# The low halves of the first layer's weights: a ScalarE write and an adding transfer in place of a VectorE subtraction

## The chip, the core and the metric

One Trainium2 chip, one of its cores. The metric is the device time in microseconds (us) of one launch. The core has TensorE (matrix products), VectorE and ScalarE (elementwise work), GpSimd (elementwise work, and the issue of indirect and adding transfers), SyncE (here it only issues transfers) and 16 DMA engines that all queues share. Each engine has its own instruction stream and runs it in order; a semaphore wait in it holds up everything behind it.

## The reference, cut to what matters

Attention over chunks gives `x` of 3072 tokens by 512. Then come two layers of eight experts, each with weights `w1` (512 x 1024) and `w2` (1024 x 512) in float32:

```python
def _moe_ref(x, w_gate, w1, w2):            # first layer
    cap = N // E                            # 384 tokens for each expert
    order = np.argsort(-(x @ w_gate).flatten())
    ...                                     # best pairs first; an expert closes when it has cap tokens
    for e in range(E):
        mask = assigned == e
        h = np.maximum(x[mask] @ w1[e], 0.0)
        out[mask] = h @ w2[e]

def _moe2_ref(x, w_gate, w_noise, noise, w1, w2):   # second layer
    ...                                     # two experts for each token, softmax over their two logits
    for e in range(E):
        for k in range(2):
            mask = top2[:, k] == e
            h = np.maximum(x[mask] @ w1[e], 0.0)
            out[mask] += top2_w[mask, k, None] * (h @ w2[e])
```

## The kernel before

TensorE multiplies operands of type fp32r, which keep fewer bits than float32. So each factor is split in two: a high half, the value rounded to fp32r, and a low half, value minus high half, rounded too. A product is the sum of three passes, high x high, high x low and low x high (`PASSES`). Weights are split in the core: `w1_sb` and `w2_sb` hold the raw weights of one expert, `w1_part[0]`, `w2_part[0]` the high halves and `[1]` the low halves.

An expert's weights are cut into eight parts `c` of 512 KB, four of `w1` (0 to 3) and four of `w2` (`CH` + 0 to `CH` + 3, that is 4 to 7). For each part and each turn (0 to 7: the eight experts of the first layer; 8, called E: the first expert of the second layer; from 9 on: the tiles of the second) four things happen:

- SyncE loads the raw part (`load_weights`, L474; in the second layer L495) once the low half of the part's previous turn has been written (`lo_ready`).
- ScalarE writes the high half (`w_high`, L530), when the raw part is there (`w_loaded`) and TensorE has finished with the part's last turn (`wait_used`).
- VectorE writes the low half (`w_low`, L536): `raw - high`, 128 x 1024 elements.
- TensorE waits for `hi_ready` and `lo_ready` ahead of the first product that uses the part (L726, L747).

There is one raw buffer, so the next load of a part waits for the low half.

The launch has four stages. Attention lasts to about 230 us. In the first expert layer (230 to 686 us) step `n` chooses the tokens of the `n`-th expert to be filled (a search in seven rounds `s` for a threshold: VectorE compares, L1115; TensorE counts, L682 and L689; VectorE reads the count, L1143 and L1164), and in its gaps the code written out by hand runs the experts before: for `k = n - 1` the token numbers are worked out (L1068 to L1071), GpSimd gathers its 384 rows (`xg`, three indirect transfers, L356, then three of noise, L360), TensorE transposes them (`turn_xg`, L696) and does its first products (`hidden`, L730); for `j = n - 2` TensorE does the rest of `hidden` and the second products (`combine`, L750), ScalarE copies the result out (`copy_y`, L1446) for a store and a transpose (`turn_y`, L704). Steps 0 to 6 choose; steps 7, 8 and 9 only finish the experts left. A routing stage (686 to 729 us) is a chain of small VectorE instructions that plans the second layer. The second layer runs 29 tiles of 256 rows to the end.

The order on ScalarE in a step is: the last `s1_high` (L1435) of the step before, `w_high` of parts 6 and 7, two `s1_high`, `w_high` 0 and 1, `copy_y` 0, `w_high` 2 and 3, `copy_y` 1, the copies of `xg`, `w_high` 4, `copy_y` 2, `w_high` 5, then `s1_high` of the next expert. VectorE's `w_low` stand at L1130 and L1159 (parts 6 and 7), L1139 and L1161 (0 to 3), L1184 and L1204 (4 and 5), and L1382 for turn E.

## Time and profile before

| | us |
|---|---|
| Median of 3 runs (lowest to highest) | 1428.52 (1428.26 to 1435.44) |
| The profiled execution, its own time | 1426.65 |
| Its span, first to last instruction | 1424.9 |
| Of that: first expert layer | about 230 to 686 |
| Routing stage | 686 to 729 |
| Second layer | 729 to the end |

Times in rows of the trace are microseconds from the start of the span. PE is TensorE (PEld its weight loads), DVE VectorE, ACT ScalarE, POOL GpSimd, SP SyncE. In a timeline, a row is start, duration, engine, line, operation, output and inputs, count, and in brackets the idle time before it with what ended it.

### The profile page before, as it was taken

The numbers are of one execution on the slowest core, as the hardware profiler recorded it, in microseconds if no ns is written. First come the engines' busy times: TensorE is split into PE (matmuls) and PEld (weight loads), VectorE is DVE, ScalarE is ACT, GpSimd is POOL, SyncE is SP. The second block draws the span as 40 slices with busy tenths as digits, with TensorE's granted clock in tenths as the row PEclk, the third lists the DMA queues.
The fourth block names the chain that finished last, engine by engine and source line by source line (L and its number), as shares of the span: only waits on it lengthen the run. The fifth ranks groups of instructions, "written<-read, shape, count | busy, mean of one in ns | idle before, by whom it ended". The sixth has DMA issues, their size and how long they took to land.

```text
span 1424.9 us, 28417 instructions
## 1 busy us (share of the span) xinstructions
PE 1268.4 (89%) x9825; PEld 1125.7 (79%) x9825; DVE 952.5 (67%) x1904; ACT 594.2 (42%) x1252; POOL 294.3 (21%) x345
## 2 busy tenths in 40 slices
PE   7999962599989999889249999999999999999997
PEld 6888851478778778768149999898989999999996
DVE  4777757788888787344666666666666666666662
ACT  4666621123323323333214545444445454444541
POOL 2000000210220210220122423332323333333322
PEclk9999975599999999899659999999999999999999
DMA  8888853133333233432013425124343324252110
GB/s 144 169 161 166 169 199 120 57 123 115 102 111 113 88 123 115 144 133 72 16 46 104 133 60 177 38 82 134 94 147 117 131 81 138 72 163 87 61 32 3
DMA packets 174760, 154.62 MB, mean 109 GB/s; under 512 B 105581, under 2 KB 138349, under 8 KB 174704
## 3 DMA queue, kind: packets, MB, share of 16 engines
q1 hardware_dynamic: 151552, 102.83, 26.2%
q0 software_dynamic: 16608, 44.56, 10.1%
q10 hardware_dynamic: 6544, 6.49, 1.3%
q8 instruction: 35, 0.57, 0.2%
q14 instruction: 21, 0.17, 0.0%
HBM read 215.58 MB, written 34.28 MB: 175 GB/s over the span
## 4 chain that ended last, share of the span: by engine, by line
issue 38%; PE 31%; DVE 12%; POOL 10%; DMA 6%; ACT 2%; POOLq 1%; DVEq 0%; SPq 0%; ACTq 0%
PE bank L730 6%; PE bank L750 5%; POOL partial L400 3%; DMA out<-result,token_now 3%; PE bank L612 3%; POOL out L404 3%; DMA xg<-x_dram,token_of 3%; PE bank L621 2%; PE bank L600 2%; POOL held L382 2%; PE bank L682 2%; POOL x L386 2%; PE bank L636 2%; PE bank L696 1%; PE bank L629 1%
## 5 line engine op out<-in xcount | busy, mean ns | idle before, releaser
L536 DVE TENSOR_TENSOR w_part<-w_sb,w_part 128x1024 fp32r<-128x1024 f32 x296 | 361.1, 1223 | 113.8 <-ACT w_part L530 105.4
L530 ACT CAST w_part<-w_sb 128x1024 fp32r<-128x1024 f32 x296 | 307.0, 1046 | 215.1 <-PE bank L890 169.7
L873 PEld LDWEIGHTS bank<-x2T,w_part 128*128 128x128 f32 x2784 | 339.2, 193 | 4.0 <-DVE x2T L1332 1.8
L873 PE MATMUL bank<-x2T,w_part 128*128 128x256 f32 x2784 | 340.1, 284 | 1.4 <-DVE x2T L1332 1.4
L890 PE MATMUL bank<-w_part,h2T 128*128 128x512 f32 x1392 | 323.2, 391 | 0.0
L890 PEld LDWEIGHTS bank<-w_part,h2T 128*128 128x128 f32 x1392 | 259.2, 188 | 52.6
L750 PE MATMUL bank<-w_part,hT 128*128 128x512 f32 x576 | 155.3, 409 | 8.2 <-DVE w_part L536 8.2
L730 PE MATMUL bank<-xgT,w_part 128*128 128x384 f32 x768 | 146.4, 345 | 2.6 <-DVE hT L1040 1.8
L356 POOL DMA_INDIRECT xg<-x_dram,token_of x24 | 32.6, 1358 | 554.9 <-DVE token_of L1071 302.5
L1544 ACT ACTIVATE h2T<-bank 128x512 fp32r<-128x512 f32 x116 | 69.3, 597 | 174.8 <-PE bank L873 174.8
L730 PEld LDWEIGHTS bank<-xgT,w_part 128*128 128x128 f32 x768 | 135.8, 192 | 5.0 <-DVE hT L1040 1.6
L1338 DVE SCALAR_TENSOR_TENSOR h2T<-bank,h2T 128x512 fp32r<-128x512 f32 x116 | 80.2, 692 | 86.0 <-ACT h2T L1544 86.0
L750 PEld LDWEIGHTS bank<-w_part,hT 128*128 128x128 f32 x576 | 103.4, 190 | 28.1 <-issue 9.7
L382 POOL TENSOR_TENSOR held<-iota_p 1x1 f32<-1x1 f32 x87 | 41.3, 475 | 406.7 <-DVE result L1357 388.3
L1392 ACT ACTIVATE probs<-bank,neg_max 96x128 f32<-96x128 f32 x256 | 89.3, 368 | 7.9 <-DVE neg_max L909 7.9
L1435 ACT ACTIVATE hT<-bank 128x384 fp32r<-128x384 f32 x64 | 31.5, 492 | 126.6 <-PE bank L730 126.6
L1357 DVE SCALAR_TENSOR_TENSOR result<-bank,w_now,partial 128x512 f32<-128x512 f32 x58 | 43.4, 748 | 44.8 <-PE bank L890 44.8
L386 POOL DMA_INDIRECT x<-y_dram,slot_now x58 | 60.9, 1050 | 56.0 <-DVE slot_now L1324 38.6
L682 PEld LDWEIGHTS bank<-above,proposal 128*8 128x8 bf16 x1176 | 31.8, 83 | 51.1 <-DVE above L1115 44.1
L682 PE MATMUL bank<-above,proposal 128*8 128x32 bf16 (+1 forms) x1176 | 37.5, 177 | 38.8 <-DVE above L1115 38.8
L400 POOL DMA_INDIRECT partial<-out,token_now x58 | 62.5, 1078 | 18.6 <-issue 16.2
L404 POOL DMA_INDIRECT out<-result,token_now x58 | 59.2, 1021 | 21.6 <-POOL held L382 16.0
(256 smaller groups left out, 1341.9 us busy)
## 6 DMA issues: line engine op xcount, KB each, us to landing
w_sb<-in_moe_w SPq DMA_DIRECT2D x296, 512.0 KB
k_in<-in_k SPq DMA_DIRECT2D x32, 240.0 KB
v_in<-in_v SPq DMA_DIRECT2D x32, 240.0 KB
q_in<-in_q SPq DMA_DIRECT2D x32, 192.0 KB
x_dram<-x_sb SPq DMA_DIRECT2D x32, 192.0 KB, 3.4
out<-zeros SPq DMA_DIRECT2D x1, 6144.0 KB, 19.7
y_dram<-y_sb ACTq DMA_DIRECT2D x24, 256.0 KB, 2.0
x<-y_dram,slot_now POOLq DMA_INDIRECT x58
```

Source lines behind the costliest of these rows:

```text
L386: pool.indirect_dma_start(out=x2[:, par, half, :], out_offset=None, in_=y_dram[:, :], in_offset=bass.IndirectOffsetOnAxis(ap=slot_now[:, p ...
L400: pool.indirect_dma_start(out=partial[:, par, half, :], out_offset=None, in_=out[:, :], in_offset=tokens[half], bounds_check=N - 1, oob_is ...
L404: pool.indirect_dma_start(out=out[:, :], out_offset=tokens[half], in_=result[:, par, half, :], in_offset=None, bounds_check=N - 1, oob_is_ ...
L530: scalar.copy(split_part(0, c), raw_part(c)).then_inc(hi_ready[c], 1)
L536: nc.vector.tensor_tensor(split_part(1, c), raw_part(c), split_part(0, c).bitcast(F32), ALU.subtract).then_inc(lo_ready[c], 1)
L682: last = nc.tensor.matmul(counts[:, 0:bins], proposal[:, c, :], above[:, c, 0:bins], start=(c == 0), stop=(c == COLS - 1))
L730: last = nc.tensor.matmul(bank[2 + f % 2][:, 0:CAP], w1_part[a][:, kt, f * P:(f + 1) * P], xgT[b][:, kt, :], start=(kt == 0 and n == 0), s ...
L750: last = nc.tensor.matmul(bank[4 + t % 2][:, :], hT[a_][:, f, t * P:(t + 1) * P], w2_part[b_][:, f, :], start=(f == 0 and n == 0), stop=(f ...
L873: last = nc.tensor.matmul(bank[2 + g % 2][:, at:at + TILE], w1_part[a][:, kt, f * P:(f + 1) * P], x2T[b][:, kt, :], start=(f % 2 == 0 and ...
L890: last = nc.tensor.matmul(bank[4 + half][:, :], h2T[a][:, f, half * P:(half + 1) * P], w2_part[b][:, f, :], start=(f == 0 and n == 0), sto ...
L1338: V.scalar_tensor_tensor(h2T[1][:, two_f, :].rearrange("p k s -> p (k s)"), bank[2 + g % 2][:], 0.0, h2T[0][:, two_f, :].bitcast(F32).rear ...
L1392: nc.scalar.activation(probs[:, r, j, :], ps_s[r][0:QB, j * P:(j + 1) * P], ACT.Exp, bias=neg_max[:, r, j:j + 1], accum_out=row_sum[:, i % ...
```

## The change

For turns 0 to E, thus for 9 x 8 = 72 parts, VectorE's subtraction is gone. ScalarE writes, right behind each high half, the negated high half by multiplying the raw part by -1.0 with the low-half tile of type fp32r as output (the same rounding, other sign; `minus_ready`). GpSimd then issues a transfer from the raw tile to the low-half tile that adds (`w_low_add`, `accum_op=ALU.add`; `lo_added`). So the tile ends as raw minus high, as before. The loads of SyncE and the products of TensorE wait for `lo_added`. In GpSimd's stream the adds of parts 0 to 3 of turn `e` stand ahead of the gathers of expert `e`, those of parts 4 to 7 behind its noise gathers; for turn E they stand behind the loop and behind the two clears of `x2` and `partial`. The second layer's other turns keep VectorE's subtraction; its counts now start from 0, so that the first of the tiles is told apart (`reload`, `wait_low`). The helpers `wait_used`, `raw_part`, `split_part`, `w_high` and `w_low` are moved up in the file, unchanged but for the lines below. Blank lines are left out here.

```diff
@@ -284,6 +284,8 @@
         o_done = sem("o_done")
         token_ready = sem("token_ready")
         hi_ready = [sem(f"hi_ready{c}") for c in range(2 * CH)]
+        minus_ready = [sem(f"minus_ready{c}") for c in range(2 * CH)]
+        lo_added = [sem(f"lo_added{c}") for c in range(2 * CH)]
         lo_ready = [sem(f"lo_ready{c}") for c in range(2 * CH)]
         part_used = [sem(f"part_used{c}") for c in range(2 * CH - 1)]
         h_hi = sem("h_hi")
@@ -299,6 +301,43 @@
 
             eng.wait_ge(tiles_ready, 1)
             return eng.value_load(pairs_i[0:1, 0:1], min_val=2 * N // TILE // 2 - 1, max_val=(TILES - 3) // 2)
+        FC = F // CH
+        def wait_used(eng, turn, c, layer):
+            if isinstance(turn, int) and turn == 0:
+                return
+            if c < 2 * CH - 1:
+                eng.wait_ge(part_used[c], turn)
+            elif layer == 1:
+                eng.wait_ge(y_ready, TPE * turn)
+            else:
+                eng.wait_ge(o_ready, 2 * (turn - E))
+        def raw_part(c):
+            return w1_sb[:, :, c * FC:(c + 1) * FC] if c < CH else w2_sb[:, (c - CH) * FC // P:(c - CH + 1) * FC // P, :]
+        def split_part(side, c):
+            return w1_part[side][:, :, c * FC:(c + 1) * FC] if c < CH else w2_part[side][:, (c - CH) * FC // P:(c - CH + 1) * FC // P, :]
+        def w_high(turn, c, layer):
+            scalar = nc.scalar
+            scalar.wait_ge(w_loaded[c], 16 * (turn + 1))
+            wait_used(scalar, turn, c, layer)
+            scalar.copy(split_part(0, c), raw_part(c)).then_inc(hi_ready[c], 1)
+            if layer == 1:
+                scalar.mul(split_part(1, c), raw_part(c), -1.0).then_inc(minus_ready[c], 1)
+        def w_low(turn, c, layer):
+            wait_used(nc.vector, turn, c, layer)
+            nc.vector.wait_ge(hi_ready[c], turn + 1)
+            nc.vector.tensor_tensor(split_part(1, c), raw_part(c), split_part(0, c).bitcast(F32), ALU.subtract).then_inc(lo_ready[c], 1)
+        def w_low_add(turn, c):
+            nc.gpsimd.wait_ge(minus_ready[c], turn + 1)
+            nc.gpsimd.dma_start(split_part(1, c), raw_part(c), accum_op=ALU.add).then_inc(lo_added[c], 16)
 
         @block.gpsimd
         def _(pool):
@@ -348,6 +387,8 @@
 
 
             for e in range(E):
+                for c in range(CH):
+                    w_low_add(e, c)
                 pool.wait_ge(tokens_ready, e + 1)
                 if e:
 
@@ -360,6 +401,10 @@
                     pool.indirect_dma_start(out=noise_g[:, c, :], out_offset=None, in_=moe2_noise[:, :],
                                             in_offset=bass.IndirectOffsetOnAxis(ap=token_of[:, c:c + 1], axis=0),
                                             bounds_check=N - 1, oob_is_err=False).then_inc(noise_in, 16)
+                for c in range(CH, 2 * CH):
+                    w_low_add(e, c)
+            for c in range(CH):
+                w_low_add(E, c)
 
 
             pool.wait_ge(g2_copied, E * TPE)
@@ -368,6 +413,8 @@
             nc.gpsimd.memset(x2[:], 0.0).then_inc(x2_cleared, 1)
             nc.gpsimd.memset(partial[:], 0.0).then_inc(x2_cleared, 1)
             pool.wait_ge(x2_cleared, 2)
+            for c in range(CH, 2 * CH):
+                w_low_add(E, c)
 
 
             pool.wait_ge(tiles_ready, 1)
@@ -469,7 +516,7 @@
             def load_weights(e, w1, w2, turn):
                 for c in range(2 * CH):
                     if not (isinstance(turn, int) and turn == 0):
-                        sp.wait_ge(lo_ready[c], turn)
+                        sp.wait_ge(lo_added[c], 16 * turn)
                     raw, src = weight_part(w1, w2, e, c)
                     sp.dma_start(raw, src).then_inc(w_loaded[c], 16)
 
@@ -486,13 +533,20 @@
 
             load_weights(0, moe2_w1, moe2_w2, E)
             sp.wait_ge(tiles_ready, 1)
-            with sp.Fori(1, 2 * tile_pairs(sp) + 3) as j:
+            def reload(j):
                 e = sp.value_load(expert_i[0:1, bass.ds(j, 1)], min_val=0, max_val=E - 1)
                 changed = sp.value_load(change_i[0:1, bass.ds(j, 1)], min_val=0, max_val=1)
                 for c in range(2 * CH):
-                    sp.wait_ge(lo_ready[c], E + j)
+                    if isinstance(j, int):
+                        sp.wait_ge(lo_added[c], 16 * (E + 1))
+                    else:
+                        sp.wait_ge(lo_ready[c], j - 1)
                     raw, src = weight_part(moe2_w1, moe2_w2, e, c)
                     sp.dma_start(raw, src, cond=changed).then_inc(w_loaded[c], 16)
+            reload(1)
+            with sp.Fori(2, 2 * tile_pairs(sp) + 3) as j:
+                reload(j)
 
         def tiles(eng, tile, pairs):
 
@@ -502,41 +556,6 @@
                 tile(2 * g + 2, 0, True, g + 1)
             tile(2 * pairs + 1, 1, True, pairs)
             tile(2 * pairs + 2, 0, False, pairs + 1)
...
         def expert_steps(eng, step):
             step(0, True, None, None)
@@ -724,7 +743,7 @@
                     pe.wait_ge(s1_lo, e * FT + f - 1)
                 if f % 2 == 0:
                     pe.wait_ge(hi_ready[f // 2], e + 1)
-                    pe.wait_ge(lo_ready[f // 2], e + 1)
+                    pe.wait_ge(lo_added[f // 2], 16 * (e + 1))
                 for kt in range(KT):
                     for n, (a, b) in enumerate(PASSES):
                         last = nc.tensor.matmul(bank[2 + f % 2][:, 0:CAP], w1_part[a][:, kt, f * P:(f + 1) * P], xgT[b][:, kt, :],
@@ -745,7 +764,7 @@
                         pe.wait_ge(s1_lo, e * FT + f + 1)
                         if f % 2 == 0:
                             pe.wait_ge(hi_ready[CH + f // 2], e + 1)
-                            pe.wait_ge(lo_ready[CH + f // 2], e + 1)
+                            pe.wait_ge(lo_added[CH + f // 2], 16 * (e + 1))
                     for n, (a_, b_) in enumerate(PASSES):
                         last = nc.tensor.matmul(bank[4 + t % 2][:, :], hT[a_][:, f, t * P:(t + 1) * P], w2_part[b_][:, f, :],
                                                 start=(f == 0 and n == 0), stop=(f == FT - 1 and n == 2))
@@ -858,6 +877,13 @@
                             last = nc.tensor.transpose(bank[pair][:, at:at + P], x2[:, par, half, kt * P:(kt + 1) * P], ident[:])
                     last.then_inc(x2_turned, 1)
 
+            def wait_low(j, c):
+                if isinstance(j, int) and j == 0:
+                    pe.wait_ge(lo_added[c], 16 * (E + 1))
+                else:
+                    pe.wait_ge(lo_ready[c], j)
             def tile(j, par, more, pair_no):
                 pe.wait_ge(x_lo, 2 * j + 2)
                 for g in range(CH):
@@ -865,7 +891,7 @@
 
                         pe.wait_ge(h_lo, CH * j + g - 1)
                     pe.wait_ge(hi_ready[g], E + j + 1)
-                    pe.wait_ge(lo_ready[g], E + j + 1)
+                    wait_low(j, g)
                     for f in (2 * g, 2 * g + 1):
                         at = (f % 2) * TILE
                         for kt in range(KT):
@@ -885,7 +911,7 @@
                         if half == 0 and f % 2 == 0:
                             pe.wait_ge(h_lo, CH * j + f // 2 + 1)
                             pe.wait_ge(hi_ready[CH + f // 2], E + j + 1)
-                            pe.wait_ge(lo_ready[CH + f // 2], E + j + 1)
+                            wait_low(j, CH + f // 2)
                         for n, (a, b) in enumerate(PASSES):
                             last = nc.tensor.matmul(bank[4 + half][:, :], h2T[a][:, f, half * P:(half + 1) * P], w2_part[b][:, f, :],
                                                     start=(f == 0 and n == 0), stop=(f == FT - 1 and n == 2))
@@ -1084,9 +1110,7 @@
                 link(V.tensor_scalar(fill_f[:], marked, -1.0, float(E), ALU.mult, ALU.add))
                 V.tensor_copy(fill_i[:, bass.ds(n, 1)], fill_f[:]).then_inc(fill_known, 1)
 
-            def step(n, route, k, j, wk=None):
-                if wk is None:
-                    wk = k
+            def step(n, route, k, j):
                 if route:
 
                     link(V.tensor_tensor(work[:], logits[:], over_cols(limit[:]), ALU.min))
@@ -1127,7 +1151,6 @@
                             s1_low(j, 5)
                         if s == 1:
                             s1_low(j, 6)
-                            w_low(j, CH + 2, 1)
                     if k is not None:
                         if s == 1:
                             taken_tiles(k)
@@ -1135,8 +1158,6 @@
                             taken_rows(k, 0)
                         if s == 6 and route:
                             xg_low(k, 1)
-                    if wk is not None and s in (3, 4, 5):
-                        w_low(wk, (0, 1, 3)[s - 3], 1)
                     if route:
                         dve.wait_ge(counts_up, n * len(SHIFTS) + s + 1)
 
@@ -1156,9 +1177,6 @@
                             xg_low(k, 2)
                     if j is not None and s == 1:
                         s1_low(j, 7)
-                        w_low(j, CH + 3, 1)
-                    if wk is not None and s == 4:
-                        w_low(wk, 2, 1)
                     if route:
                         dve.wait_ge(votes_up, n * len(SHIFTS) + s + 1)
                         link(V.tensor_scalar(votes[:, 1:bins], votes_ps[:, 1:bins], 1.0 if s == 0 else float(1 << shift), 0.0,
@@ -1181,7 +1199,6 @@
                 if k is not None:
                     for kt in (3,) if route else range(KT):
                         xg_low(k, kt)
-                    w_low(k, CH, 1)
                 if route:
 
                     dve.wait_ge(tally_up, n + 1)
@@ -1201,7 +1218,6 @@
                     link(V.scalar_tensor_tensor(room[:], filled[:], CLOSED, et[3][:], ALU.mult, ALU.add))
                     link(V.scalar_tensor_tensor(limit[:], filled[:], -3e38, limit[:], ALU.mult, ALU.add))
                 if k is not None:
-                    w_low(k, CH + 1, 1)
                     s1_low(k, 0)
                     s1_low(k, 1)
                 if route:
@@ -1238,7 +1254,7 @@
             step(E - 1, False, E - 2, E - 3)
             step(E, False, E - 1, E - 2)
 
-            step(E + 1, False, None, E - 1, E)
+            step(E + 1, False, None, E - 1)
 
 
             dve.wait_ge(g2_copied, E * TPE)
@@ -1378,8 +1394,6 @@
 
             for t in range(TPE):
                 dve.wait_ge(y_stored[t], 16 * E)
-            for c in range(CH, 2 * CH):
-                w_low(E, c, 1)
             meta(0, 0, 0, False)
             x_low(0)
             tiles(dve, tile, tile_pairs(dve))
```

## Rows read from the trace of the kernel before

**Rows 1.** Part 1 of the page: busy time and share of each engine.
```profile
PE 1268.4 (89%) x9825; PEld 1125.7 (79%) x9825; DVE 952.5 (67%) x1904; ACT 594.2 (42%) x1252; POOL 294.3 (21%) x345
```

**Rows 2.** Groups by line, 280 to 700 us: busy, mean ns, idle before.
```profile
L536 DVE TENSOR_TENSOR w_part<-w_sb,w_part 128x1024 fp32r<-128x1024 f32 x63 | 76.1, 1219 | 3.9 <-ACT w_part L530 3.1
L530 ACT CAST w_part<-w_sb 128x1024 fp32r<-128x1024 f32 x66 | 66.3, 1045 | 4.4 <-ACT y_sb L1446 4.4
```

**Rows 3.** Sums of waits, 280 to 700 us: total, times, longest.
```profile
PE bank L696 <- DMA xg<-x_dram,token_of: 8.6, 7, 2.3
PE bank L750 <- DVE w_part L536: 8.2, 8, 1.4
```

**Rows 4.** The chain that ended last, ends of one selection step: start, duration.
```profile
448.71 0.97 DVE above L1115
...
503.16 0.97 DVE above L1115
```

**Rows 5.** Timeline of TensorE, same step: start, duration, idle before.
```profile
458.90 1.55 PE L750 MATMUL bank<-w_part,hT 128*128 128x512 f32 x6
...
461.46 1.62 PE L750 MATMUL bank<-w_part,hT 128*128 128x512 f32 x6 [0.89 <-DVE w_part L536]
...
476.99 0.76 PE L682 MATMUL bank<-above,proposal 128*8 128x32 bf16 x24 [1.00 <-DVE above L1115]
478.76 0.54 PE L696 MATMUL bank<-ident,xg 128*128 128x128 f32 x3 [1.01 <-DMA xg<-x_dram,token_of]
...
488.92 0.66 PE L704 MATMUL bank<-ident,y_sb 128*128 128x128 f32 x4
```

**Rows 6.** Timeline of ScalarE, same step.
```profile
449.86 1.99 ACT L530 CAST w_part<-w_sb 128x1024 fp32r<-128x1024 f32 x2
...
459.48 1.98 ACT L530 CAST w_part<-w_sb 128x1024 fp32r<-128x1024 f32 x2
...
464.30 2.00 ACT L530 CAST w_part<-w_sb 128x1024 fp32r<-128x1024 f32 x2 [0.60 <-ACT y_sb L1446]
...
487.33 1.05 ACT L530 CAST w_part<-w_sb 128x1024 fp32r<-128x1024 f32 x1
488.28 0.59 ACT L1446 COPY y_sb<-bank 128x512 f32<-128x512 f32 x1
```

**Rows 7.** Timeline of VectorE, same step.
```profile
460.09 1.22 DVE L536 TENSOR_TENSOR w_part<-w_sb,w_part 128x1024 fp32r<-128x1024 f32 x1
```

**Rows 8.** Timeline of GpSimd, same step: issues of the first two gathers.
```profile
471.36 1.00 POOL L356 DMA_INDIRECT xg<-x_dram,token_of  x1 [44.34 <-DVE token_of L1071]
472.66 1.99 POOL L356 DMA_INDIRECT xg<-x_dram,token_of  x1 [0.30 <-issue]
```

**Rows 9.** Line 356 (gathers): issue to landing.
```profile
DMA to landing us min/median/max: 3.7/4.2/8.6
```

**Rows 10.** Stage 500 to 504 us: length, busy times, clock, DMA share, GB/s.
```profile
500.00:504.00 4.00, 3.88 (x24) 3.34 (x23) 3.76 (x9) 0.58 (x2) 0.00 (x0) 1.00 1.05 373
```

**Rows 11.** Timeline of TensorE, first step without a selection.
```profile
565.12 1.55 PE L750 MATMUL bank<-w_part,hT 128*128 128x512 f32 x6
568.03 2.96 PE L750 MATMUL bank<-w_part,hT 128*128 128x512 f32 x12 [1.35 <-DVE w_part L536]
...
584.34 0.55 PE L696 MATMUL bank<-ident,xg 128*128 128x128 f32 x3 [2.00 <-DMA xg<-x_dram,token_of]
```

**Rows 12.** Timeline of ScalarE, same step as rows 11.
```profile
558.76 1.99 ACT L530 CAST w_part<-w_sb 128x1024 fp32r<-128x1024 f32 x2
...
569.73 0.59 ACT L1446 COPY y_sb<-bank 128x512 f32<-128x512 f32 x1 [2.03 <-PE bank L750]
```

**Rows 13.** Timeline of VectorE, start of the second layer.
```profile
728.64 4.63 DVE L536 TENSOR_TENSOR w_part<-w_sb,w_part 128x1024 fp32r<-128x1024 f32 x4
```

**Rows 14.** Timeline of GpSimd, start of the second layer: second gather.
```profile
731.05 1.96 POOL L386 DMA_INDIRECT x<-y_dram,slot_now  x1 [0.30 <-issue]
```

**Rows 15.** Timeline of TensorE, start of the second layer.
```profile
735.48 1.97 PE L858 MATMUL bank<-ident,x 128*128 128x128 f32 x8 [8.58 <-DMA x<-y_dram,slot_now]
```

More of the change, by code:

```diff
@@ L504, in tiles @@
             tile(2 * pairs + 2, 0, False, pairs + 1)
-        FC = F // CH
-        def wait_used(eng, turn, c, layer):
-            if isinstance(turn, int) and turn == 0:
-                return
-            if c < 2 * CH - 1:
-                eng.wait_ge(part_used[c], turn)
-            elif layer == 1:
-                eng.wait_ge(y_ready, TPE * turn)
-            else:
-                eng.wait_ge(o_ready, 2 * (turn - E))
-        def raw_part(c):
-            return w1_sb[:, :, c * FC:(c + 1) * FC] if c < CH else w2_sb[:, (c - CH) * FC // P:(c - CH + 1) * FC // P, :]
-        def split_part(side, c):
-            return w1_part[side][:, :, c * FC:(c + 1) * FC] if c < CH else w2_part[side][:, (c - CH) * FC // P:(c - CH + 1) * FC // P, :]
-        def w_high(turn, c, layer):
-            scalar = nc.scalar
-            scalar.wait_ge(w_loaded[c], 16 * (turn + 1))
-            wait_used(scalar, turn, c, layer)
-            scalar.copy(split_part(0, c), raw_part(c)).then_inc(hi_ready[c], 1)
-        def w_low(turn, c, layer):
-            wait_used(nc.vector, turn, c, layer)
-            nc.vector.wait_ge(hi_ready[c], turn + 1)
-            nc.vector.tensor_tensor(split_part(1, c), raw_part(c), split_part(0, c).bitcast(F32), ALU.subtract).then_inc(lo_ready[c], 1)
         def expert_steps(eng, step):
```

## Prediction

> **What bounds the kernel now.** I read part 1 of the page first [rows 1]: TensorE is busy for 89% of the span, VectorE for 67%. The change touches only the first expert layer and the two seams behind it, so the rest is left alone; the groups and sums of waits from 280 to 700 us come next [rows 2, 3]. VectorE's low halves cost 1.22 us each, and of the 63 in that stretch only 8 had TensorE waiting, 8.2 us in all. The gathers of `xg` made it wait as long: 8.6 us. So the 72 removed instructions (72 x 1.22 = 88 us of VectorE) are not 88 us of the end. A selection step lasts 54.45 us [rows 4], and its TensorE timeline shows three gaps near this work [rows 5]: 0.89 us ahead of the products at 461.46, for the low half of part 7; 1.00 us ahead of the count at 476.99, for a compare that VectorE reached late; 1.01 us ahead of the transposes at 478.76, for the gathers. TensorE is nearly full and the gathers are the next limit. What the step can win is under 3 us, and what the step can lose is whatever makes part 6, part 7 or the gathers later.
>
> **What goes away.** VectorE's low half of part 7 ran from 460.09 [rows 7] and its end freed TensorE. Without it the products need only `s1_low`, and could start 0.9 us sooner, if the added half is there. In the steps without selection the gap is 1.35 us [rows 11]. The late compare (1.00 us) also goes, but behind it TensorE meets the gathers in order, so that gap moves into the wait for them. It is worth something only if the gathers come sooner. They could: the second gather's issue took 1.99 us where the first took 1.00 [rows 8], at the same time as low halves on VectorE, and the same is seen where the second layer starts: 1.96 us [rows 14] during four low halves in a row [rows 13].
>
> The Trainium skill, page SBUF — State Buffer, section "Who interferes with whom", says that a VectorE instruction with two SBUF inputs contends with a GpSimd instruction that reads SBUF. By that the longer issues are those under the subtractions, as seen here; the sum is the same without it.
>
> **What ScalarE adds.** 72 multiplications of the size of the cast, which takes 1.045 us [rows 2]: 75 us on an engine with much room. A multiplication of this shape is not in the trace; below, nothing of its size is cheaper than 0.59 us for 512 columns [rows 6], above, I see no reason for more than the cast. I take 1.0 us. Most lie in idle time. One place does not: `copy_y` 2 stands directly behind `w_high` 4, at 488.28 for 0.59 us, and TensorE's transpose that needs it starts at 488.92 with no gap [rows 5, 6]. One more microsecond ahead of it is a microsecond of TensorE: +0.95 us in each of the five steps that select and finish an expert (steps 2 to 6). In steps 7 and 8 `copy_y` 2 comes ahead of `w_high` 4, cost nothing there.
>
> **What an add costs.** No add is in the trace. It moves 524,288 bytes. Weight loads, at full share of the DMA engines, move 373 GB/s [rows 10]: 1.4 us for a part. An add must read the raw half and the tile and write the tile. From below: 1.4 us, if both reads overlap. From above: nothing bounds an adder's rate, so I take twice the doubled load, 5.6 us. The value taken is two reads at the load's rate, 2.8 us. Around it: a gather of 256 KB takes 3.7 us from issue to landing [rows 9], of which 0.7 us is data at 373 GB/s, so 3.0 us is fixed; the release of GpSimd costs some 0.7 us (the gathers' token numbers against the issue at 471.36 [rows 8]). An add lands about 0.7 + 3.0 + 2.8 = 6.5 us after its minus half, and adds in a row land 2.8 us apart.
>
> The Trainium skill, page Collectives: The Full Stack, section "The bandwidth ceiling: the fold count and why AG ≠ RS ≠ AR", says that an adding transfer needs two source reads on the same ring and so runs at half the rate of a copy, not because the adder costs cycles. By that an add is 2.8 us of data, as taken, and the 5.6 us bound would be out; no row here shows it.
>
> The issue itself: GpSimd spends 1.00 us on a gather of 128 rows [rows 8]. A part of `w2` is 128 contiguous runs of 4 KB, so I take 1.0 us. A part of `w1` is 512 runs of 1 KB: from below 1.0 us, from above four times, 4.0 us. I take 2 us, as part of a gather's microsecond is fixed.
>
> **Parts 6 and 7.** High halves 6 and 7 start at 449.86 [rows 6]; with a minus half behind each, minus 6 ends near 451.9 and minus 7 near 453.9. Add 6 lands at 458.4; TensorE needs it at 458.90 [rows 5]. Add 7 lands at 461.2, or 461.9 with the load of part 6 beside it; now the products start at 461.46. So the 0.9 us is not won: +0.5 us instead. In step 7 the pair starts at 558.76 [rows 12], minus 6 ends at 560.8, add 6 lands at 567.3, needed at 565.12; add 7 lands at 570.1 against 568.03 now [rows 11]: about +2.2 us, likewise in steps 8 and 9.
>
> **Parts 0 to 3 against the gathers.** The pair at 459.48 becomes four instructions to 463.5; `copy_y` 0 and then the pair now at 464.30 follow, so minus 3 ends near 468.6 [rows 6]. Add 0 starts to move at about 463.2; four adds at 2.8 us end at 474.4, with part 7's load (1.4 us) and the store of `y` (0.7 us) beside them at 476.5. The gathers are issued by the same engine, behind the adds: at best from 471.4, with their data behind the adds'. 3 x 0.7 us of data and some 1.2 us of completion put the landing near 480, against 478.7 now: +1.4 us, and the won compare doesn't show. In steps 7 and 8 `copy_y` 0 waits until 569.73 [rows 12], or some 2 us more with the delay above; two high and two minus halves behind it end near 577, and GpSimd cannot issue the gathers (now 573 to 578) before. They land at about 586.3 against 584.34 [rows 11]; the 2.2 us from parts 6 and 7 lies inside the same wait. I take +1.8 us.
>
> **The seams.** In the routing stage, GpSimd issues the last four adds while VectorE runs its chain of small instructions; I allow +1 us (from nothing to 4 us, one for each issue). At the start of the second layer VectorE's four low halves go [rows 13]. They held up no product, since TensorE waits for the rows of `x` until 735.48 [rows 15], but the gather's issue beside them took 1.96 us instead of 1.00 [rows 14]: -1.3 us with the first one's share. If the cover were gone, they would be 4.63 us of path. Parts 4 and 5, and step 1, have time enough.
>
> **Sum.** Steps 2 to 6: 0.95 + 0.5 + 1.4 = 2.9, times 5 = 14.3. Steps 7 and 8: 2 x 1.8 = 3.6. Step 9 (no gathers): 2.2. Seams: +1.0 - 1.3. Together +19.8 us on the profiled execution's own 1426.65 (span 1424.9), thus 1446; that execution is 1.9 us under the median of the runs, so 1448 on the median.
>
> **Rivals.**
> A. The adds are slow, in the engines or in their issue. With 4 us for the issue of each `w1` part, GpSimd is free for the gathers at 462.2 + 4 x 4.3 = 479.4 instead of 471.4: +8 us in a step, seven times, less 1.4 already counted: about +46, 1494. With 5.6 us of data, four adds end at 463.2 + 22.4 + 2.1 = 487.7, the gathers land at 491, +12.5 us in a step: 1525. For it: nothing in the trace prices an add. Against: 1 us for 128 rows.
> B. The other side: the adds are cheap (landing within 4.5 us of the minus half, data under 1.8 us each, which lets four of them end before 471.4), and the relief counts: 8.2 us of waits on low halves [rows 3], one of the 1.0 us gaps in each of seven steps for the earlier gathers (7), 1.3 at the seam, against 0.95 x 5 on ScalarE: -11.7, 1417. It decides between 1.8 and 2.2 us of data for an add. For it: at 1.4 us (both reads overlapping) it holds.
> C. All transfers are hidden but the gains are eaten: part 7 and the gathers land as now, ScalarE costs 4.75, the seam returns 1.3, waits on low halves fall by half (-4): 1428.
> D. The change doesn't move the work: adds fall back on few DMA engines. Then each takes several times 2.8 us; it ends in A.
>
> **Numbers.** My forecast (faster adds than A, slower than B; 1436 to 1465) 0.38, A and D together 0.25, B 0.20, C 0.17. The range reaches from B to most of A: 1418 to 1498. 0.5% is 7 us, what a measurement of this kernel can tell from none: faster 0.20, same 0.19, slower 0.61.
>
> **What would show it.** Right: adds some 5 to 7 us from issue to landing; new waits of TensorE at L750 for a transfer into `w_part`; at L696 longer waits for the gathers; `turn_y` waiting about 1 us for `copy_y`; the second gather's issue back at 1.0 us. Wrong: adds landing in under 4.5 us (B); POOL issues of `w1` parts over 3 us, or the DMA engines full from 461 us through the gathers (A); a minus half much longer than 1.05 us.

## The result and the profile after

| | before | changed |
|---|---|---|
| Median, us (lowest to highest) | 1431.98 (1428.26 to 1445.84) | 1482.35 (1478.88 to 1485.54) |
| Span of the profiled execution, us | 1424.9 | 1482.5 |
| Mean granted clock of TensorE | 0.940 | 0.915 |

The ratio is 1.0345, 95% interval 1.0315 to 1.0376: the change makes the kernel 3.5% slower. Slower was forecast, but 20 us of it. The medians differ by 50.4 us and the spans of the two profiled executions by 57.6 us; the ledger below is of the spans.

Part 3 of the page of before has for the queue of GpSimd's transfers (packets, MB, share of 16 engines):

```profile
q0 software_dynamic: 16608, 44.56, 10.1%
```

The page of the changed kernel, parts 1, 3, 5 and 6:

```profile
PE 1291.6 (87%) x9825; PEld 1144.4 (77%) x9825; DVE 875.6 (59%) x1832; ACT 660.9 (45%) x1324; POOL 366.6 (25%) x417
...
q0 software_dynamic: 40800, 82.31, 25.6%
...
L340 POOL DMA_DIRECT2D w_part<-w_sb x72 | 78.4, 1090 | 578.7 <-ACT w_part L331 578.5
...
L331 ACT ACTIVATE w_part<-w_sb 128x1024 fp32r<-128x1024 f32 x72 | 76.1, 1057 | 0.0
...
w_part<-w_sb POOLq DMA_DIRECT2D x72, 512.0 KB, 6.5
```

The 72 writes of ScalarE take 1.057 us, as priced, and GpSimd spends 1.09 us on an add's issue in the mean (0.85 us for a part of `w2`, 1.28 us for one of `w1` in the rows below), where I had taken 1 and 2 us. An add takes 6.5 us from issue to landing in the median; 3.0 + 2.8 = 5.8 was forecast. In the DMA engines it costs (0.256 x 1482.5 - 0.101 x 1424.9) / 72 = 3.27 us of all sixteen in the mean, not 2.8.

That mean hides two kinds. From 472 to 483 us queue q0 carries two adds of `w2` and nothing else, at 52.8% of the 16 engines: 11 x 0.528 / 2 = 2.9 us each, as forecast. From 484 to 506 us it carries four adds of `w1` and six gathers, at 80.2%, which is 17.6 us; the same six gathers took 3.4 us before (21.1% from 470 to 486 us). That leaves 14.2 / 4 = 3.6 us for an add of `w1`, whose runs are 1 KB instead of 4 KB. These are the ones ahead of the gathers.

The waits of TensorE from 230 to 800 us, first that of before and then two of the changed kernel, and the gathers' way from issue to landing:

```profile
PE bank L696 <- DMA xg<-x_dram,token_of: 11.1, 8, 2.5
...
PE bank L715 <- DMA xg<-x_dram,token_of: 49.3, 8, 9.5
...
PE bank L769 <- DMA w_part<-w_sb: 5.8, 6, 1.6
```

```profile
DMA to landing us min/median/max: 3.6/9.0/12.5
```

The gathers are the place: 49.3 us of waits where the same kind was 11.1 us (8.6 of it in the stretch of [rows 3]), and a median of 9.0 us to land against 4.2 [rows 9]. The waits for low halves went from 8.2 us [rows 3] to 5.8.

The same selection step as in rows 4 to 8, now between these two pieces of the chain (start, duration):

```profile
471.77 0.97 DVE above L1139
...
532.79 0.97 DVE above L1139
```

TensorE's timeline in it, then GpSimd's, then two stages of it (length, busy times, clock, DMA share, GB/s):

```profile
481.98 1.55 PE L769 MATMUL bank<-w_part,hT 128*128 128x512 f32 x6
...
483.57 1.65 PE L769 MATMUL bank<-w_part,hT 128*128 128x512 f32 x6
...
498.95 0.75 PE L701 MATMUL bank<-above,proposal 128*8 128x32 bf16 x24 [0.48 <-DVE above L1139]
505.35 0.90 PE L715 MATMUL bank<-ident,xg 128*128 128x128 f32 x3 [5.64 <-DMA xg<-x_dram,token_of]
...
518.91 0.66 PE L723 MATMUL bank<-ident,y_sb 128*128 128x128 f32 x4 [0.17 <-ACT y_sb L1460]
```

```profile
484.85 1.29 POOL L340 DMA_DIRECT2D w_part<-w_sb  x1 [6.90 <-ACT w_part L331]
...
491.81 1.28 POOL L340 DMA_DIRECT2D w_part<-w_sb  x1 [0.25 <-ACT w_part L331]
494.52 1.40 POOL L397 DMA_INDIRECT xg<-x_dram,token_of  x1 [1.44 <-issue]
496.23 1.07 POOL L397 DMA_INDIRECT xg<-x_dram,token_of  x1 [0.30 <-issue]
```

```profile
488.00:502.00 14.00, 11.23 (x132) 8.26 (x132) 7.27 (x25) 4.69 (x6) 8.52 (x9) 1.00 1.15 184
506.00:514.00 8.00, 8.00 (x53) 6.47 (x52) 2.30 (x9) 1.85 (x5) 0.00 (x0) 0.50 0.00 0
```

The step is 61.02 us long instead of 54.45 [rows 4], and three sections of it, with [rows 5], say where the 6.6 us are:

- Up to the count of round 5 it is faster: 498.95 - 471.77 = 27.2 us against 28.3. The products of part 7 start at 483.57 with no wait; the 0.89 us is won.
- From that count to the first transpose of the gathered rows: 6.4 us against 1.8, so +4.6. The adds of parts 0 to 3 are issued from 484.85 to 491.81, and between 488 and 502 us the DMA engines are full (share 1.15; the packets' times are added up, so overlapping ones can pass 1). The gathers, issued from 494.52 on, stand behind them. Their issue is not late: the first starts 22.75 us after the start of the step, 22.65 before [rows 4, 8]. All of the delay lies between issue and landing.
- From there to the transposes of `y` at 518.91: 13.6 us against 10.2, so +3.4, with the same instructions in it. After 5.64 us of idle TensorE, the granted clock is 0.50 from 506 to 514 us, the lower of its two levels (1.2 of 2.4 GHz), and everything takes longer: the three transposes at 505.35 took 0.90 us, 0.54 before.

The rest of the step is 0.4 us shorter. Counted from the start of the step, the gathers are 3.5 us late (4.6 less the 1.1 won ahead of them). Step 7, the first without a selection (TensorE, then GpSimd):

```profile
602.54 1.64 PE L769 MATMUL bank<-w_part,hT 128*128 128x512 f32 x6 [0.47 <-DMA w_part<-w_sb]
605.46 2.98 PE L769 MATMUL bank<-w_part,hT 128*128 128x512 f32 x12 [1.28 <-DMA w_part<-w_sb]
...
627.57 0.90 PE L715 MATMUL bank<-ident,xg 128*128 128x128 f32 x3 [7.78 <-DMA xg<-x_dram,token_of]
```

```profile
597.84 0.85 POOL L340 DMA_DIRECT2D w_part<-w_sb  x1 [12.95 <-ACT w_part L331]
599.73 0.85 POOL L340 DMA_DIRECT2D w_part<-w_sb  x1 [1.05 <-ACT w_part L331]
...
612.43 1.28 POOL L340 DMA_DIRECT2D w_part<-w_sb  x1 [0.63 <-ACT w_part L331]
614.02 1.10 POOL L397 DMA_INDIRECT xg<-x_dram,token_of  x1 [0.30 <-issue]
```

The gathers' wait is 7.78 us where it was 2.00 [rows 11]. Part 3's add holds the first gather's issue until 614.02, and part 7's add lands 1.28 us late.

The ledger of the 57.6 us, by the same events in both traces: steps 1 to 5 +29.6, steps 6 to 9 +25.9, routing stage +2.5, the fetch at the start of the second layer -1.2, the second layer +0.7. (Rounded; steps 2 to 5 alone are +6.3, +7.3, +9.7 and +6.6.)

### The profile page after: what moved, and what is told of

Its sections match the earlier page's. It is cut to its first block, busy times and chain, and to the rows that moved or that the text cites. A ratio compares the mean times of both kernels' runs of the same rounds, so it can differ in the third digit from the quotient of the medians.

```text
span 1482.5 us, 28430 instructions
## 1 busy us (share of the span) xinstructions
PE 1291.6 (87%) x9825; PEld 1144.4 (77%) x9825; DVE 875.6 (59%) x1832; ACT 660.9 (45%) x1324; POOL 366.6 (25%) x417
## 4 chain that ended last, share of the span: by engine, by line
issue 36%; PE 32%; POOL 9%; DVE 9%; DMA 9%; ACT 3%; POOLq 1%; SPq 0%; ACTq 0%; DVEq 0%
PE bank L749 7%; PE bank L769 5%; DMA xg<-x_dram,token_of 5%; DMA out<-result,token_now 3%; PE bank L631 3%; POOL partial L447 3%; POOL out L451 3%; PE bank L640 2%; PE bank L619 2%; POOL held L429 2%; PE bank L715 2%; POOL x L433 2%; PE bank L701 2%; PE bank L655 2%; PE bank L734 1%
## 5 line engine op out<-in xcount | busy, mean ns | idle before, releaser
L336 DVE TENSOR_TENSOR w_part<-w_sb,w_part 128x1024 fp32r<-128x1024 f32 x224 | 274.3, 1225 | 110.7 <-ACT w_part L329 103.1
L340 POOL DMA_DIRECT2D w_part<-w_sb x72 | 78.4, 1090 | 578.7 <-ACT w_part L331 578.5
L769 PE MATMUL bank<-w_part,hT 128*128 128x512 f32 x576 | 165.6, 428 | 5.8 <-DMA w_part<-w_sb 5.8
L1354 DVE SCALAR_TENSOR_TENSOR h2T<-bank,h2T 128x512 fp32r<-128x512 f32 x116 | 80.2, 692 | 86.7 <-ACT h2T L1558 86.7
L769 PEld LDWEIGHTS bank<-w_part,hT 128*128 128x128 f32 x576 | 109.4, 202 | 27.3 <-issue 7.9
L715 PE MATMUL bank<-ident,xg 128*128 128x128 f32 x96 | 27.5, 422 | 57.7 <-DMA xg<-x_dram,token_of 49.3
L1062 DVE TENSOR_TENSOR xgT<-bank,xgT 128x384 fp32r<-128x384 f32 x32 | 17.8, 556 | 100.4 <-ACT xgT L1445 100.4
L331 ACT ACTIVATE w_part<-w_sb 128x1024 fp32r<-128x1024 f32 x72 | 76.1, 1057 | 0.0
L1066 DVE SCALAR_TENSOR_TENSOR hT<-bank,hT 128x384 fp32r<-128x384 f32 x64 | 35.2, 556 | 60.2 <-ACT hT L1449 58.9
```

Of the source, the lines that this page charges most:

```text
L331: scalar.mul(split_part(1, c), raw_part(c), -1.0).then_inc(minus_ready[c], 1)
L336: nc.vector.tensor_tensor(split_part(1, c), raw_part(c), split_part(0, c).bitcast(F32), ALU.subtract).then_inc(lo_ready[c], 1)
L340: nc.gpsimd.dma_start(split_part(1, c), raw_part(c), accum_op=ALU.add).then_inc(lo_added[c], 16)
L769: last = nc.tensor.matmul(bank[4 + t % 2][:, :], hT[a_][:, f, t * P:(t + 1) * P], w2_part[b_][:, f, :], start=(f == 0 and n == 0), stop=(f ...
L1354: V.scalar_tensor_tensor(h2T[1][:, two_f, :].rearrange("p k s -> p (k s)"), bank[2 + g % 2][:], 0.0, h2T[0][:, two_f, :].bitcast(F32).rear ...
```

## The experiments

My theory behind the result: the adds are not slow in themselves. They fill the DMA engines just ahead of the gathers, so TensorE waits, and the wait costs its clock too. Rivals: the sum of the traffic or ScalarE's longer queue, wherever they stand; an adder that is slow; the wait alone, with the clock only a sign of it.

**gathers_first.** One order in GpSimd's stream:

```diff
             for e in range(E):
-                for c in range(CH):
-                    w_low_add(e, c)
                 pool.wait_ge(tokens_ready, e + 1)
...                                             (the three gathers of xg)
+                for c in range(CH):
+                    w_low_add(e, c)
...                                             (the three gathers of noise)
```

> Same work as the changed kernel, one order changed: GpSimd issues the three gathers of an expert ahead of the adds of parts 0 to 3. Theory (the adds fill the DMA engines just ahead of the gathers, and the late gathers cost TensorE a wait and then its clock): the waits of TensorE for the gathers fall from 49 us to about 10, the granted clock returns to about 0.94, and the time falls by 40 to 55 us, to 1425 to 1442. Rival (the price is the sum of the added DMA traffic or ScalarE's longer queue, wherever they stand): not below 1465.

Measured: 1427.53 us, ratio 0.9965 (0.9948 to 0.9983). The same 72 adds, multiplications and bytes, and all 3.5% are gone. Its waits for the gathers (230 to 800 us), and TensorE in the step:

```profile
PE bank L715 <- DMA xg<-x_dram,token_of: 8.2, 6, 2.4
```

```profile
481.01 0.54 PE L715 MATMUL bank<-ident,xg 128*128 128x128 f32 x3 [1.39 <-DMA xg<-x_dram,token_of]
...
491.05 1.11 PE L723 MATMUL bank<-ident,y_sb 128*128 128x128 f32 x4 [0.85 <-ACT y_sb L1460]
```

8.2 us instead of 49.3. The rival falls: traffic and ScalarE's queue are unchanged. The second row shows a price that was forecast and hardly showed in that step of the changed kernel: 0.85 us for `copy_y` 2, which stands behind the added write of part 4. It too has the clock behind it. The mean granted clock is 0.61 from 491 to 495 us, and the next 24 products take 5.48 us, 4.42 before the change:

```profile
491.81 5.48 PE L749 MATMUL bank<-xgT,w_part 128*128 128x384 f32 x24
```

**two_ahead.** The adds of parts 0 and 1 stay ahead of the gathers, 2 and 3 go behind.

```diff
-                for c in range(CH):
+                for c in range(CH // 2):
                     w_low_add(e, c)
                 pool.wait_ge(tokens_ready, e + 1)
...
+                for c in range(CH // 2, CH):
+                    w_low_add(e, c)
```

> The changed kernel with the adds of parts 0 and 1 ahead of the gathers and those of 2 and 3 behind them. Theory (the gathers are late only by what the DMA engines still owe when they are issued; two adds of 3.7 us are worked off by then): the wait for the gathers stays about 10 us, time within 5 us of the kernel with all four behind, 1423 to 1435. Rival (each add ahead costs its share): half of the loss, 1450 to 1460.

Measured: 1433.60 us, ratio 0.9979 (0.9956 to 1.0002). The waits for the gathers:

```profile
PE bank L717 <- DMA xg<-x_dram,token_of: 6.0, 6, 2.4
```

Two adds ahead cost nothing that can be told from none ahead, four cost 50 us. So there is no fixed price for each add; what fits is a queue that is worked off in time or is not.

**copy.** A plain transfer in place of the adding one, and a small high half to keep the products' size:

```diff
-            scalar.copy(split_part(0, c), raw_part(c)).then_inc(hi_ready[c], 1)
+            scalar.mul(split_part(0, c), raw_part(c), 1e-4).then_inc(hi_ready[c], 1)   # turns 0 to E
...
-            nc.gpsimd.dma_start(split_part(1, c), raw_part(c), accum_op=ALU.add).then_inc(lo_added[c], 16)
+            nc.gpsimd.dma_start(split_part(1, c), raw_part(c)).then_inc(lo_added[c], 16)
```

> The transfers copy the raw part over the low half instead of adding to it (one read in place of two); the high half of these turns is 0.0001 x raw, so that the products stay of the same size. Theory (an add costs what two reads cost): a transfer takes about 1.7 us of the 16 engines instead of 3.3, the wait for the gathers falls to about 15 us, time 1435 to 1450. Rival (the software queue or a cast is slow, not the second read): transfers still take about 3 us each and the time stays over 1470.

Measured: 1432.46 us, ratio 1.0000 (0.9983 to 1.0017). Its page, parts 3, 5 and 6, and its waits for the gathers:

```profile
q0 software_dynamic: 40800, 82.31, 19.3%
...
L343 POOL DMA_DIRECT2D w_part<-w_sb x72 | 47.0, 652 | 562.0 <-ACT w_part L334 558.4
...
w_part<-w_sb POOLq DMA_DIRECT2D x72, 512.0 KB, 3.5
...
PE bank L718 <- DMA xg<-x_dram,token_of: 16.7, 8, 4.0
```

A copy costs (0.193 x 1431.6 - 0.101 x 1424.9) / 72 = 1.84 us of the engines, an add 3.27, 1.78 times as much, and lands in 3.5 us instead of 6.5. The difference, 1.43 us, is what one read of a part at the load's rate would take (1.4 us), so a second read accounts for it; no run separates that read from the adding itself. With little over half the cost ahead of them the gathers cost 16.7 us of waits, and the loss is gone. The Trainium skill, page Collectives: The Full Stack, section "The bandwidth ceiling: the fold count and why AG ≠ RS ≠ AR", says this of the reduce step of a ring between cores: its adding transfers need two source reads and so run at half the rate of copies. Here, inside one core, 1.78 is near that factor of two.

**no_transfer.** No add at all; the low half of turns 0 to E is left at 0.0001 x raw, so the true low halves are missing from the products:

```diff
-                scalar.mul(split_part(1, c), raw_part(c), -1.0).then_inc(minus_ready[c], 1)
+                scalar.mul(split_part(1, c), raw_part(c), 1e-4).then_inc(minus_ready[c], 1)
...                                             (w_low_add returns at once; lo_added waits become minus_ready waits)
```

> The adding transfers are left out; ScalarE writes 0.0001 x raw into the low half instead of minus the raw part, and loads and products wait for that write. So VectorE's relief and ScalarE's 72 writes are there without a transfer. Theory: 1416 to 1426, faster than the kernel before, by the waits on low halves that are gone (8 us) and earlier gathers, less about 5 us on ScalarE. Rival (ScalarE's longer queue is a large part of the 50 us): 1440 or more.

Measured: 1420.98 us, ratio 0.9919 (0.9892 to 0.9945). This is what the relief of VectorE is worth without a transfer and with ScalarE's longer queue, 0.8%. ScalarE's price stands in TensorE's timeline here too:

```profile
488.36 1.11 PE L722 MATMUL bank<-ident,y_sb 128*128 128x128 f32 x4 [0.85 <-ACT y_sb L1459]
```

**w2_only.** Parts 4 to 7 by minus half and add, 0 to 3 by VectorE's `w_low` at its old places.

```diff
-            if layer == 1:
+            if layer == 1 and c >= CH:
                 scalar.mul(split_part(1, c), raw_part(c), -1.0).then_inc(minus_ready[c], 1)
...                                             (waits of parts 0 to 3 on lo_ready again, their adds gone)
+                    if wk is not None and s in (3, 4, 5):
+                        w_low(wk, (0, 1, 3)[s - 3], 1)
```

> Only parts 4 to 7 are made by ScalarE and the adding transfer; parts 0 to 3 are subtracted on VectorE where they stood before. Theory: no add stands ahead of a gather any more, wait for gathers about 9 us as before, what is left is ScalarE ahead of copy_y 2 (+5) and late parts 6 and 7 in the last three steps (+1 to +5): 1425 to 1440. Rival (every add costs the same, wherever it stands): half of the 50 us, about 1455.

Measured: 1435.70 us, ratio 1.0011 (0.9980 to 1.0042). With half of the adds there, but none just ahead of a gather, nothing is lost. TensorE waits 13.1 us for the gathers, not the 9 that I expected; no single wait is over 2.4 us.

**filler.** Is the clock a cost of its own? Products of constants fill the wait (the wait for `gathered`, shown last, also moves behind that for `xg_lo`):

```diff
+                if kt == 0:
+                    for i in range(30):
+                        nc.tensor.matmul(bank[0][:, 0:3 * P], ones[:], window[:].rearrange("p k s -> p (k s)"), start=True, stop=True)
                 pe.wait_ge(gathered, 16 * TPE * (e + 1))
```

> The changed kernel, and ahead of the first transpose of each expert's gathered rows TensorE runs 30 more products of constants (128 x 384, bf16, some 0.17 us each, thus 5 us that fit in the wait of 5.6 to 9.5 us) into a bank that the transposes overwrite. Gathers, adds and all waits stay as they are. Theory (part of the loss is TensorE's clock, which falls to half in the wait and stays there for some 12 us behind it): the granted clock stays 1.00 behind the wait in the selecting steps, some 3 us a step come back, time 1456 to 1470. Rival (the wait alone is the loss, the clock is a sign of it): 1480 or more.

Measured: 1477.05 us, ratio 1.0262 (1.0226 to 1.0299), against 1.0345 (1.0315 to 1.0376). The same step in its trace: TensorE, and the stage behind the wait:

```profile
499.61 5.05 PE L715 MATMUL bank<-window,ones 128*128 128x384 bf16 x30
505.17 0.55 PE L718 MATMUL bank<-ident,xg 128*128 128x128 f32 x3 [0.52 <-DMA xg<-x_dram,token_of]
```

```profile
506.00:514.00 8.00, 7.29 (x82) 5.89 (x81) 4.81 (x19) 3.56 (x8) 0.00 (x0) 1.00 0.00 0
```

The gathers land at the same time, 505.2, the clock stays at 1.00, the transposes take 0.55 us, and the step lasts 58.67 us instead of 61.02. So the lower clock costs on its own. From the first transposes to the transposes of `y` that `copy_y` 2 frees it is 10.05 us instead of 13.56.

The median is outside the 1456 to 1470 that I expected, and the trace shows why:

- Where there is no long wait, as in the first gather's step, 30 products are pure work (that step is 53.06 us long instead of 49.67).
- The products don't always fit the wait. In step 3 the clock had already fallen to 0.50 when they ran; they took 6.47 us, and the transposes waited for them and no longer for the gathers. In step 7 they end 3.93 us before the gathers land, and the clock behind is 0.50 again. So steps 2 and 3 are 1.0 and 0.8 us longer than in the changed kernel, steps 4 and 5 are 5.1 and 2.4 us shorter.
- With the full clock `copy_y` 2's wait of 0.85 us comes out from under the slow stretch and brings one of its own: 0.50 from 516 to 518 us.

How much the clock takes of the whole loss stays open. The filler wins back 5.3 us by the medians, 6.0 by the spans and 12 by the two ratios, whose before medians differ by 4.7 us. From above, seven waits of over 5 us with 3.4 us behind each are an estimate of 24 us.

**gathers_first_y.** `gathers_first`, with part 4's minus half behind `copy_y` 2 in the selecting steps:

```diff
                     copy_y(j, 2)
                     copy_gate(j, 1)
+                    if k is not None and route:
+                        nc.scalar.mul(split_part(1, CH), raw_part(CH), -1.0).then_inc(minus_ready[CH], 1)
```

> The order of gathers_first, and in the selecting steps ScalarE writes the minus half of part 4 behind copy_y 2 instead of ahead of it. Theory (the 0.85 us wait of TensorE ahead of the transposes of y is ScalarE's added write): that wait goes in the five steps, 4 to 7 us faster than gathers_first, 1420 to 1424. Rival (the microsecond is hidden or reappears at the next wait): within 1.5 us of gathers_first.

Measured: 1430.11 us, ratio 0.9956 (0.9939 to 0.9972). That is not told apart from `gathers_first`; the 4 to 7 us that I expected did not come. In the profile of the step the 0.85 us is gone, and two smaller gaps stand ahead of it:

```profile
486.60 0.17 PE L711 MATMUL bank<-met,ones 8*128 8x4 bf16 x1 [0.61 <-DVE met L1167]
487.50 0.55 PE L718 MATMUL bank<-ident,xg 128*128 128x128 f32 x3 [0.73 <-DVE xgT L1065]
```

So most of the microsecond is won there (steps 3 to 5 take 53.4 to 53.6 us against 54.4 to 55.5), but step 2 took 55.79 us against 52.42, and the time doesn't show it.

**The clears.** The routing stage lost 2.5 us, and 1.8 us in `no_transfer` and `gathers_first`. In the changed kernel, VectorE and GpSimd at that place:

```profile
742.09 1.89 DVE L1266 TENSOR_SCALAR z_abs<-z_exp 128x192 f32<-128x192 f32 x1 [0.43 <-ACT z_exp L1540]
744.02 1.82 DVE L1267 COPY work<-z_abs 128x192 f32<-128x192 f32 x1
```

```profile
742.01 1.86 POOL L413 MEMSET x<- 128x2112 f32 x1 [10.41 <-DMA y_dram<-y_sb]
```

Two one-input instructions of 128 x 192 take 1.89 and 1.82 us, exactly as long as GpSimd's clears stand beside them. The stores of `y` set when the clears start, and any change of the steps ahead moves them. In `gathers_first` they start with the stage, and other instructions stand beside them: the first of the stage (L1262) takes 2.00 us and L1266 takes 1.03 us, while L1267 takes 0.26. `gathers_first_clear` and `gathers_first_y_clear` are the two versions above with one line:

```diff
+            pool.wait_ge(log_up, 1)
             nc.gpsimd.memset(x2[:], 0.0).then_inc(x2_cleared, 1)
```

> gathers_first with one wait more: GpSimd clears x2 and partial only when ScalarE's logarithm is done (log_up). Theory (the clears stand beside two one-input instructions of VectorE, which then take 1.89 and 1.82 us instead of 0.26 each): those two are back at 0.26 us, the routing stage is some 2.5 us shorter, 1.5 to 3 us faster than gathers_first against the same runs of before (ratio 0.994 to 0.996). Rival (they were slow for another reason, or the stage waits elsewhere): ratio 0.9965 as gathers_first.

> gathers_first_y with the same wait for the clears. Theory: ratio 0.992 to 0.995, the best of the versions, TensorE's wait for the copy of y gone and the routing stage 2.5 us shorter. If the order of the minus half of part 4 brings nothing, it equals gathers_first_clear.

Measured: 1427.04 us, ratio 0.9950 (0.9927 to 0.9972), and 1423.26 us, ratio 0.9939 (0.9914 to 0.9964). VectorE and GpSimd of `gathers_first_clear`:

```profile
687.68 0.26 DVE L1267 TENSOR_SCALAR z_abs<-z_exp 128x192 f32<-128x192 f32 x1 [0.43 <-ACT z_exp L1541]
687.98 0.26 DVE L1268 COPY work<-z_abs 128x192 f32<-128x192 f32 x1
```

```profile
689.47 1.86 POOL L414 MEMSET x<- 128x2112 f32 x1 [12.28 <-ACT z_log L1543]
```

Both instructions take 0.26 us, and the stage takes 42.9 us in both clear versions as before the change, where it was 44.7 us in `gathers_first`: shown in the profile. In the time, 0.9950 against 0.9965 is inside both intervals. The Trainium skill, page SBUF — State Buffer, section "Who interferes with whom", has it that a VectorE copy or one-input operation in its two-port mode and a GpSimd instruction shut each other out for a whole instruction; the rows agree. `gathers_first_y_clear` beats both kernels, by 0.6% the one before; it is not told apart from the other two.

## Why the prediction was wrong, point by point

The sign, the place and the mechanism were right: the adds ahead of the gathers. The size was not: 20 us against 50.4 between the medians and 57.6 between the spans. The step that failed is "Parts 0 to 3 against the gathers", in two terms.

- **The backlog was undersized.** I had the gathers land 17.8 us after the first add's issue (462.2 to 480); it was 20.5 (484.85 to 505.35). The adds of `w1` take 3.6 us each where 2.8 stood, 3.2 us for four. The loads and the store of `y` beside them take 3.4 us from 484 to 506 us (7.3% and 8.3% of 22 us) where 2.1 stood. Together that is more than the 2.7 us, so part of it overlaps. The 1.2 us of completion in the same sum had no row behind it. In front of a wait with no slack left, the excess shows: the gathers are 3.5 us late in this step instead of 1.4, and in steps 7 and 8 TensorE waits 7.8 and 9.5 us, where +1.8 was summed on the 2.00 of before.
- **The clock was left out.** Behind each of these waits TensorE works at the lower level for a while, +3.4 us in this step. No term and no rival had it, though the trace before has it at smaller size: 0.50 from 480 to 482 us, behind the waits of 1.00 and 1.01 us in [rows 5]. `filler` shows it is a cost of its own.
- **Rival A** gave nearly the right time (1494) for the wrong reason. Its 4 us for the issue of a `w1` part was measured at 1.28, its 5.6 us in the engines at 3.6. Of its signs one did come, the DMA engines full ahead of and through the gathers: adds of 3.6 us are enough for that, so the sign does not tell A from my forecast.
- **Parts 6 and 7** were overpriced. I forecast +0.5 us in a selecting step and +2.2 in the last one (in steps 7 and 8 inside the gathers' wait; in the selecting steps I added both terms, though the same holds there). Measured: the 0.89 us won in the first, and waits of 0.47 + 1.28 us in step 7 where 1.35 stood. The adds of these parts landed 4.7 and 5.7 us after their issue at 597.84 and 599.73, earlier than the 5.8 and one behind the other that I had taken.
- **ScalarE ahead of `copy_y` 2:** right in mechanism, 0.85 us for 0.95, in `gathers_first`, `no_transfer` and `filler`. In the step shown of the changed kernel only 0.17 us shows, as TensorE itself was slow there; over all steps it waited 2.1 us for `y_sb` against 4.4 in `gathers_first`. The lower clock behind this wait was in no term either.
- **The gather's issue:** right. The second gather's issue took 1.07 us (was 1.99, [rows 8]), though the first took 1.40 (was 1.00), and the fetch before the second layer is 1.2 us shorter (1.3 forecast).
- **The routing stage:** +2.5 for +1, and not by the adds' issues but by the clears.
- **Rival B** (the relief counts) was true as a bound: `no_transfer` gives 0.8%, 1421, where I had worked out 1417. With four adds of 3.27 us ahead of the gathers it had no chance; with the order changed, 0.35% could be had, and 0.6% with the two further changes.

## What to carry to other kernels

Before work is moved to the DMA engines, ask which transfer that an engine will wait for is issued next on the same queue, and add up all that the engines owe at that moment; with the order changed, the same adds cost nothing. Price a transfer by its own run length, not by a load's rate: here 1 KB runs cost a quarter more than 4 KB runs of the same bytes. A wait on TensorE has to be priced with the lower clock behind it, here another 3.4 us on 4.6. If a long queue cannot be avoided, put the transfer that somebody waits for ahead of it and those with slack behind. Not tested is whether the gathers suffer from standing behind the adds on their own queue or from the full engines alone: all adds and gathers here share one queue, and no run puts the traffic on another.

## What the runs showed of the hardware

- An adding transfer of 512 KB between two tiles in SBUF costs 3.27 us of the sixteen engines in the mean (2.9 us in runs of 4 KB, 3.6 us in runs of 1 KB), the same transfer as a copy 1.84 us; from issue to landing 6.5 and 3.5 us in the median. GpSimd spends 1.09 us on the issue of an add and 0.65 us on that of a copy.
- The loss does not grow in proportion to the adds ahead: with no, two and four of them ahead of the gathers the ratios to before are 0.9965, 0.9979 and 1.0345.
- Constant products that filled a wait to its last 0.52 us kept the granted clock at 1.00 behind it, where it was 0.50 without them. With 3.93 us left unfilled it was 0.50 all the same. Behind a wait of 0.85 us alone it also fell, to a mean of 0.61 over 4 us in `gathers_first`.
- GpSimd's clears of 1.86 us stretched one-input VectorE instructions beside them from 0.26 to 1.89 us.
